# The first four attention units of a fused linear-attention and expert kernel get a program of their own

## The reference

```python
def _attn_ref(r, k, v, w, u):                   # B, H, S, D = 4, 8, 768, 48
    for t in range(S):
        kt, vt, rt, wt = (k[:, :, t], v[:, :, t], r[:, :, t], w[:, :, t])
        cur = np.einsum('bhd,bhe->bhde', u[None] * kt, vt)
        y[:, :, t] = np.einsum('bhd,bhde->bhe', rt, state + cur)
        state = wt[:, :, :, None] * state + np.einsum('bhd,bhe->bhde', kt, vt)

x = y.transpose(0, 2, 1, 3).reshape(3072, 384)
h = x @ w_in                                    # 384 -> 2048
x = (h * np.clip(h + 3.0, 0.0, 6.0) / 6.0) @ w_out
logits = x @ phi                                # 32 slots, 4 for each of 8 experts
# soft mixture: slots = softmax(logits, 0).T @ x; each expert: relu(slots @ w1) @ w2;
# out = softmax(logits, 1) @ slot_out
```

## Time and profile before

| | us |
|---|---|
| median of 3 runs | 466.13 (465.29 to 466.23) |
| the profiled execution | 466.87 |
| its span, first to last instruction | 465.2 |
| first product of a unit | starts at 8.54 |
| first MLP product (s = 0) | starts at 56.84 |
| first MLP product of group 1 (s = 16) | starts at 117.76 |

### The profile page before, as it was taken

How to read it: one execution, slowest core, us unless ns; L and a number is a source line. 1 busy time by engine, 2 the same in 40 slices (tenths; PEclk the granted TensorE clock), 3 DMA queues, 4 the chain that set the end, 5 groups by cost and what they waited for, 6 DMA issues and landing times.

```text
span 465.2 us, 9561 instructions
## 1 busy us (share of the span) xinstructions
PE 429.4 (92%) x3774; PEld 228.5 (49%) x3774; DVE 358.0 (77%) x577; ACT 155.1 (33%) x277; POOL 209.1 (45%) x207
## 2 busy tenths in 40 slices
PE   2977898899999999999999999899999999999974
PEld 1544464545556555655555566355553443443420
DVE  6789989988888888988899989888875576562233
ACT  2234333443334324323435143242333222231122
POOL 5889856456652666456555455655460000000000
PEclk9989999899999999999999999999999999999975
DMA  8999333035812321332233303331006952669729
GB/s 229 277 348 345 89 111 92 20 112 191 281 30 104 111 79 46 101 112 66 54 103 112 112 4 109 110 112 54 1 1 264 408 185 94 236 260 419 306 71 336
DMA packets 16844, 70.91 MB, mean 152 GB/s; under 512 B 2080, under 2 KB 5280, under 8 KB 14752
## 3 DMA queue, kind: packets, MB, share of 16 engines
q1 hardware_dynamic: 16800, 70.30, 44.0%
HBM read 65.57 MB, written 4.72 MB: 151 GB/s over the span
## 4 chain that ended last, share of the span: by engine, by line
PE 49%; issue 21%; DVE 14%; POOL 8%; ACT 5%; DMA 1%; DVEq 0%; SPq 0%; POOLq 0%; ACTq 0%
PE hid L471 6%; PE hid L473 5%; PE hid L472 5%; PE l_ps L527 4%; DVE gated L788 4%; PE hid L489 3%; POOL att L1134 3%; DVE att L738 3%; PE sc_ps L401 3%; POOL att L1144 3%; PE hid L648 2%; PE l_ps L501 2%; PE y_ps L440 2%; POOL att L1128 2%; PE inc_ps L424 2%
## 5 line engine op out<-in xcount | busy, mean ns | idle before, releaser
L471 PE MATMUL hid<-x_split,w_split 128*128 128x512 f16 x288 | 109.9, 381 | 2.6 <-DVE x_split L761 2.6
L472 PE MATMUL hid<-x_split,w_split 128*128 128x512 f16 x288 | 109.6, 381 | 0.0
L473 PE MATMUL hid<-x_split,w_split 128*128 128x512 f16 x288 | 109.6, 380 | 0.0
L1134 POOL TENSOR_TENSOR att<-att 128x512 f16<-128x512 f32 x48 | 59.4, 1237 | 108.1 <-ACT att L993 108.1
L1027 ACT ACTIVATE relu<-hid,three 128x512 f32<-128x512 f32 x96 | 65.7, 684 | 126.7 <-PE hid L473 126.3
L788 DVE SCALAR_TENSOR_TENSOR gated<-relu,hid 128x512 f32<-128x512 f32 x96 | 65.4, 681 | 31.5 <-ACT relu L1027 31.1
L798 DVE STREAM_TRANSPOSE ring<-gated 128x512 f32<-128x512 f32 x96 | 68.3, 711 | 3.3
L993 ACT ACTIVATE att<-att 128x512 f16<-128x512 f32 x48 | 30.3, 631 | 99.0 <-DVE att L738 94.5
L401 PE MATMUL sc_ps<-att 48*128 48x128 f32 x384 | 35.8, 306 | 17.9 <-DVE att L732 8.5
L471 PEld LDWEIGHTS hid<-x_split,w_split 128*128 128x128 f16 x288 | 28.5, 99 | 40.0 <-issue 7.5
L401 PEld LDWEIGHTS sc_ps<-att 48*128 48x128 f32 x384 | 26.5, 195 | 40.6 <-issue 31.1
(11 more groups left out here) (195 smaller groups left out, 763.5 us busy)
## 6 DMA issues: line engine op xcount, KB each, us to landing
att<-nat_dram SPq DMA_DIRECT2D x22, 576.0 KB, 4.1
att<-rkT_dram SPq DMA_DIRECT2D x22, 448.0 KB, 5.5
att<-w_dram SPq DMA_DIRECT2D x5, 1536.0 KB, 14.3
att<-wT_dram SPq DMA_DIRECT2D x22, 226.2 KB, 4.7
out_dram<-w_split SPq DMA_DIRECT2D x24, 192.0 KB, 2.5
stage<-w_in_dram SPq DMA_DIRECT2D x2, 1536.0 KB, 25.1
ring<-w_outT_dram SPq DMA_DIRECT2D x1, 3072.0 KB, 30.0
stage<-w_dram SPq DMA_DIRECT2D x2, 1536.0 KB, 10.3
```

The lines of the kernel that those rows point to most:

```text
L471: pe.matmul(hid[s % 2][:], high, x_high, start=(q == 0), stop=False)
L472: pe.matmul(hid[s % 2][:], high, x_low, start=False, stop=False)
L473: last = pe.matmul(hid[s % 2][:], low, x_high, start=False, stop=(q == KT - 1))
L1134: nc.gpsimd.tensor_tensor(halves(scores_lo, half), halves(scores, half), halves(scores_hi, half), ALU.subtract).then_inc(scores_lo_done, 1)
```

## The change

The head of steps with s < 0 is gone. Each engine has a written-out program for units 0 to 3 and part of unit 4, and then the loop from s = 0.

- **Units 0 to 3:** no fp16 split of scores and v. `mask_first` masks both halves, and `attend_first` multiplies the masked fp32 scores by fp32 v: 8 products instead of 24.
- **Diagonal:** GpSimd multiplies the r and k rows once (`multiply_rows`), TensorE sums over the head dimension with u as a matrix of 2 columns (`diagonal`, 4 products), ScalarE copies the result (`copy_diag`). Units from 4 on keep the old way.
- **Loads:** of `nat`, units 0 to 3 load v alone (192 KB), in a new order below; a small array `u_blocks` is loaded beside `u`.
- **Start:** TensorE opens with 16 products of zeros. State memsets on GpSimd come after unit 0's keys and first product; the fp16 copy of the identity moves to ScalarE; `make_fold` (16 copies at s = 5) becomes 4 copies at the start.
- **Around s = 0:** unit 4's `turn_keys`, `increment`, `attend` and all of `weigh_phi` come after the first MLP step; `high_w` and `low_w` of a piece come one or two steps later. VectorE turns the product of phi at s = 3.

```diff
@@ SP
             for n in range(B):
                 load_rows(n)
-                load_nat(n)
                 if n == 0:
-                    sp.dma_start(u_all, u.rearrange("h d -> (h d)").partition_broadcast(P)).then_inc(u_in, 16)
-            load_w_in(0)
+                    sp.dma_start(u_rows[0:PD, :], u_blocks).then_inc(u_rows_in, 16)
+                load_values(n)
+                if n == 2:
+                    load_w_in(0)
             load_rows(B)
             sp.dma_start(phi_sb[:], phi).then_inc(phi_in, 16)
+            sp.dma_start(u_all, u.rearrange("h d -> (h d)").partition_broadcast(P)).then_inc(u_in, 16)
+            load_nat(B)
             sp.dma_start(w_outT_stage, w_outT).then_inc(w_outT_in, 16)
-            load_nat(B)
+            load_rows(B + 1)
+            load_nat(B + 1)
             load_w_in(1)
@@ TensorE
+            def attend_first(n):
+                if n:
+                    pe.wait_ge(x_lo_done, n)
+                pe.wait_ge(nat_in[n % B], 16)
+                for p in range(PB):
+                    if p % 2 == 0:
+                        pe.wait_ge(masked, 2 * n + p // 2 + 1)
+                    for j in range(2):
+                        cols = slice((2 * p + j) * D, (2 * p + j + 1) * D)
+                        last = pe.matmul(y_ps[:, cols], scores[:, (j * PB + p) * P:(j * PB + p + 1) * P],
+                                         nat_of(n, 2)[:, cols], start=True, stop=True, skip_group_check=True)
+                last.then_inc(y_ready, 1)
...
+            for _ in range(16):
+                pe.matmul(hid[0][:, :], warm[:, 0:P], warm[:, P:P + GT], start=True, stop=True, skip_group_check=True)
+            for half in range(2):
+                score(0, half, None)
+            pe.wait_ge(pool_consts, 2)
+            pe.wait_ge(ident16_done, 1)
+            diagonal(0)
+            for n in range(B):
+                if n:
+                    for half in range(2):
+                        score(n, half, None)
+                turn_keys(n)
+                if n + 1 < B:
+                    diagonal(n + 1)
+                else:
+                    stay_warm(2, hid[0])
+                attend_first(n)
+                increment(n, None)
+                turn_x(n)
+                stay_warm(1, hid[0])
+            for half in range(2):
+                score(B, half, None)
@@ VectorE
+            make_fold()
+            scan_suffix(0)
+            restart_prefix(0)
+            scan_prefix(0)
+            decay_receptance(0)
+            for n in range(B):
+                scan_suffix(n + 1)
+                restart_prefix(n + 1)
+                if n:
+                    low_x(n - 1)
+                mask_first(n)
+                scan_prefix(n + 1)
+                finish_y(n)
+                decay_receptance(n + 1)
+            low_x(B - 1)
+            low_w(0)
+            mask_first(B)
+            low_v(B)
+            sum_diag(B)
```

More of the change, by code:

```diff
@@ L46, with build_program @@
 LAST_INC = UNITS - B
-def build_program(nc, wT, rkT, nat_in_dram, u, w_in, w_outT, w_out, phi, w1, w2, out):
+def build_program(nc, wT, rkT, nat_in_dram, u, u_blocks, w_in, w_outT, w_out, phi, w1, w2, out):
     with ExitStack() as ctx:
@@ L204, in build_program @@
         u_in = sem("u_in")
+        u_rows_in = sem("u_rows_in")
         phi_in = sem("phi_in")
@@ L420, in increment @@
                 pe.wait_ge(nat_in[n % B], 16 * (n // B + 1))
-                if s >= FT and s % FT == 3:
+                if s is not None and s >= FT and s % FT == 3:
                     pe.wait_ge(logits_done, s // FT)
@@ L445, in attend @@
                         there = slice((2 * p + j) * D, (2 * p + j + 1) * D)
-                        pe.matmul(c, scores_hi[:, here], v_hi[n % 2][:, there], start=not from_state, stop=False,
+                        pe.matmul(c, scores_hi[:, here], v_hi[n % 2][:, there], start=False, stop=False,
                                   skip_group_check=True)
@@ L740, in mask_scores, with mask_first @@
                                         ALU.mult).then_inc(masked, 1)
+            def mask_first(n):
+                dve.wait_ge(scores_ready, 4 * n + 4)
+                if n:
+                    dve.wait_ge(y_ready, n)
+                for half in range(2):
+                    nc.vector.tensor_tensor(halves(scores, half), halves(sc_ps[:, :], half),
+                                            mask[:].rearrange("p (o n) -> p o n", o=1).broadcast_to([P, 2, 2 * P]),
+                                            ALU.mult).then_inc(masked, 1)
             def finish_y(n):
@@ L891, in _ @@
                         sum_diag(n)
+                if s == 0:
+                    gate(0)
+                    turn_gated(0)
+                    low_w(1)
+                    scan_suffix(B + 1)
+                    restart_prefix(B + 1)
                 if phase == 3:
@@ L1165, in _ @@
             nc.gpsimd.memset(ident[:], 0.0).then_inc(ident_step, 1)
-            for b in range(B):
-                last = nc.gpsimd.memset(state[b], 0.0)
-            last.then_inc(pool_consts, 1)
             pool.wait_ge(ident_step, 1)
@@ L1181, in _ @@
             nc.gpsimd.memset(three[:], 3.0 * GATE).then_inc(pool_consts, 1)
-            nc.gpsimd.tensor_copy(ident16_sb[:], ident[:]).then_inc(pool_consts, 1)
-            for s in range(FIRST, END):
+            decay_keys(0)
+            multiply_rows(0)
+            for b in range(B):
+                last = nc.gpsimd.memset(state[b], 0.0)
+            last.then_inc(state_zeroed, 1)
+            multiply_rows(1)
+            for n in range(B):
+                decay_keys(n + 1)
+                diag_values(n)
+                if n + 2 < B:
+                    multiply_rows(n + 2)
+            decay_state(B)
+            diag_products(B)
+            for half in range(2):
+                low_scores(B, half)
+            diag_values(B)
+            decay_keys(B + 1)
+            for s in range(END):
                 n, phase = unit_of(s)
-                in_head = n + 1 < HEAD
                 if phase == 0 and is_unit(n):
```

200 lines of the change are left out of this document (122 added, 78 removed).

## The result

| | before | after | forecast |
|---|---|---|---|
| median of 12 executions each | 466.51 | 461.58 | 450.1 |
| lowest to highest | 465.29 to 469.55 | 452.02 to 466.83 | 445 to 457 |
| ratio, with interval | | 0.974 [0.9708, 0.9771] | 0.966 |

The changed kernel is faster, but its executions differ by 14.8 us where those of before differ by 4.3. The ratio leaves out executions over 1.5% above the fastest of a kernel, which are 7 of the 12 after; those kept have a median of 455.21. By the ratio the change saves 2.6%, 12.1 us, where 16.0 was forecast; by the medians of all 12 it saves 4.9. So the side was right and the size was not: 5 of 12 executions lie inside the range, 7 above it.

A forecast was written before the change was run, and what follows sets the result against it. VectorE and GpSimd blocking each other were taken to bound the head, a chain the rest. Terms of -19.7, +4.5 and -0.75 gave -16.0 us, 466.87 to 450.9, median 450.1; range 445 to 457.

The forecast's parts named there:

- TensorE's part of a unit: Head, units 0 to 3: TensorE's scores, small groups and `attend_first` cost nothing unless the clock is low.
- the first rival: Head: TensorE falls to the lower clock, a unit's path gains 2.4 us, two units make 455; chance 0.17.
- Start: Head's opening: first scan at 3.5 us instead of 4.02, receptance product done at 8.05 against 8.39, almost no gain.
- Unit 0 to 1: Head: hangs on GpSimd's row products, state memsets, keys and diagonal values; receptance of unit 1 at 17.1, 9.0 us.
- `attend_first`: Units 0 to 3 on TensorE: fp32 products taken at 1.5 us, between 0.7 and 2.8.
- Loads: DMA into the head: at 226 GB/s each need is covered, by 1 to 3 us; `w_outT` in at 36 to 37.
- Loads as the bound: Rival, head: loads of values in short rows cost 4.5 us, unit 3's keys come 3 to 4 late, 454; chance 0.17.
- MLP to unit 5's mask: From first MLP product to unit 5's first mask: 12.3 us instead of 7.81, a loss of 4.5.
- Group 0: Behind unit 5's first mask: fold copies gone, phi transpose and one more `low_w` added, net -0.75 us.
- Locks hide fully: Rival, head: VectorE and GpSimd locks hidden, a unit takes 5.3 us, four units save 3 more, 447; chance 0.13.
- Slower than before: Rival: TensorE stays at 1.2 GHz into group 0, all 16 steps make about 473 us; chance 0.03.
- No gain: Rival: group 0's chain holds its dates by something other than unit 5's mask, such as weights; chance 0.02.

The follow-up runs named there:

- five more products in the lull: Changed kernel plus five padding products in unit 0, where TensorE waits for GpSimd's second row product: median 452.13 us, ratio 0.9708.
- full loads: The five and two version, with units 0 to 3 loading the whole of `nat` instead of v alone: 457.36 us, ratio 0.976.
- four behind each unit: Changed kernel with four padding products behind each of units 0 to 3 instead of one: median 456.52 us, ratio 0.9768.
- fold back: Changed kernel with the fold's 16 copies back after step 5, none at the start, one execution: first masks of units 5 and 6 18.39 us apart, not 16.64.
- changed kernel again: Changed kernel, nothing edited, run again as a control on the chip of later runs: median 454.85 us, ratio 0.9746.
- five and two: Changed kernel plus five padding products in unit 0's TensorE wait for GpSimd, and two behind each unit instead of one: median 451.58 us, ratio 0.9664.
- early memsets: The five and two version with state memsets ahead of unit 0's keys: 458.23 us with two products in unit 0's wait, 459.22 with five.
- no opening: Changed kernel without the 16 opening products of zeros on TensorE: median 455.43 us, ratio 0.9743.

## Why the prediction was right and wrong

**Side and mechanism: right.** The head before was paced by the two engines that block each other: without its padding and at half of TensorE's speed its units moved only from 9.7 to 10.1. The change took that away. With the level kept up for most of the head, the dates are those of the forecast: first MLP product at 37.4 (forecast 37.1), receptance of units 1 to 4 ready at 16.3, 22.3, 29.2 and 35.6 (17.1, 23.4, 29.2, 35.4), unit 5's first mask at 49.15 (49.4), unit 8's at 97.21 (about 97), group 1's first MLP product at 102.05 (about 102), span 449.7 (449.2). These are of the kernel with five more products in the lull, not of the changed kernel as it stands. That they fit to a few tenths is in part luck: units 1 and 2 came 0.8 and 1.1 us early, and the dip at 20 us took it back, with 6.9 us from unit 2 to unit 3 for a forecast 5.8.

**The step that failed** is the pricing of TensorE's part of a unit: "So it costs nothing unless the clock is low", and in the first rival "At the lower level a unit's path gains 1.1 on the scores and about 1.3 on attend and turn_x, 2.4". I followed a path through TensorE and never added up its whole unit. That sum is 5.70 us without a gap at the full level, next to VectorE's 5.8 in my forecast, and 10.60 at the lower one. So the new plan has two bounds at nearly the same height at 2.4 GHz, and at 1.2 GHz TensorE alone is the bound: 4.9 us more a unit, twice the 2.4 priced. In the profiled execution `attend_first` of units 0 to 3 stands at 13.19, 23.79, 34.39 and 43.58; with five products in the lull at 12.60, 18.81, 26.04 and 31.75. It loses 0.6, 5.0, 8.4 and 11.8. The first MLP product is then 49.18 - 37.44 = 11.7 us late and the span 461.6 - 449.7 = 11.9 longer. The mean clocks say the same: 0.949 over 461.6 us is 2 x 0.051 x 461.6 = 47 us at half speed, 0.982 over 449.7 us is 16; the 31 us between cost 11.9.

**The chance that failed** is 0.17 for this rival against 0.48 for the forecast. Each profile of the changed kernel or of a variant of its head has at least one stretch at the low level; in two it is only the dip at 20 us. I argued with the 57 padding products that were to go. What should have weighed more is that the padded head of before didn't hold the level either: its mean clock is 0.96, and it has a score group of 1.15 us instead of 0.71:

```profile
31.31 1.15 PE L401 MATMUL sc_ps<-att 48*128 48x128 f32 x8
```

The row at 84.30 is of a fall after 2.60 us of idle; I used it for the price, not for the chance. The rival's 455 for two units is too low as a price; that it equals the 455.21 above is luck.

**Terms, one by one.**
- *Start.* First scan at 3.58 (3.5), receptance product done at 7.8 (8.05), scores at 7.96: right.
- *Unit 0 to 1*, 9.0 on GpSimd: memsets and row product did stand ahead of the keys as forecast. The values ended at 14.46 instead of 15.2. At the full level receptance follows at 16.27 after 7.82, 8.4 us. There GpSimd was not alone: its values ended at 14.48, and `finish_y` at 14.60 waited for `attend_first`.
- *`attend_first`*, taken at 1.5 between 0.7 and 2.8: 1.96, and 3.63 at the low level.
- *Loads.* Right that they are covered, wrong in the rate: 350 to 409 GB/s from 8.5 to 37 us, not 226. `w_outT`, issued at 18.79, took 14.4 us and was in at 33.2 instead of 36 to 37. The 226 from the earlier trace rows counts only what was issued up to unit 3's `nat`. In the same 17.54 us of before the DMA engines moved more, with their share as high as here:

```profile
7.06:24.60 17.54, 14.80 (x100) 9.27 (x101) 13.63 (x18) 6.70 (x12) 13.12 (x10) 1.00 1.04 287
```

Why they move more still in the new head isn't shown. Loads as the bound (0.17): refuted for the changed kernel, real with full loads. Its 4.5 us for three loads of values should read 4.3, three times 2.3 less 0.87.
- *MLP to unit 5's mask*, 12.3: 49.15 - 37.44 = 11.7 at the full level, 60.88 - 49.18 = 11.7 in the profile of after.
- *Group 0*, -0.75: mask 5 to mask 8 takes 48.06, against 48.27 before, so -0.2. The fold's term is shown (1.75). The stretch from unit 5 to 6 is 16.64 where 17.46 - 1.72 + 0.3 = 16.0 was forecast, and 6 to 7 and 7 to 8 are 15.71 each for a forecast 15.74. The 0.6 between isn't traced to one instruction.
- *Locks hide fully* (447): not seen, no execution of the changed kernel is below 452.02. *Slower than before*: two executions, 466.66 and 466.83, reach the median of before, so the clock can eat the whole gain; the level is 1.00 in group 0 though, which is what that rival needed to fall. *No gain*: refuted, masks move with the head.

**Open.** What makes the level fall or hold isn't settled, and the lull at 11 us explains less than the experiments with padding suggest. The level rises somewhere within the 16 opening products (each takes 0.63 us at first and 0.38 at the end), not at the same date in each execution. In the two profiles of the changed kernel:

```profile
1.32 5.48 PE L577 MATMUL hid<-logits 128*128 128x512 f16 x16 [1.32 <-DVE logits L927]
```

```profile
1.32 6.21 PE L577 MATMUL hid<-logits 128*128 128x512 f16 x16 [1.32 <-DVE logits L927]
```

The shorter the opening products, so the sooner the level had risen, the sooner it fell again:

| profile | opening products, us | five in the lull | first fall, us |
|---|---|---|---|
| full loads | 4.93 | yes | 10.8 |
| four behind each unit | 5.04 | no | 11.0 |
| changed kernel | 5.48 | no | 11.9 |
| fold back | 5.80 | no | 12.6 |
| changed kernel again | 6.21 | no | 13.4 |
| five in the lull | 6.22 | yes | 20.3 |
| five and two | 6.40 | yes | 20.6 |

Only the last three have openings of like length. Among them the five products put the fall off by 7 us; with an opening of 4.93 they did not. So the rival, that the date of the rise decides much of what I put down to the lull, is untested, and it may be why executions of one kernel differ. In the two versions with early memsets the level fell at 9.8 and 9.3, inside idle of 2.61 and 2.83 us. And a fall needs no gap: besides those at 20.3 and 20.6, it came at 30.3 (no opening), 31.5 (four behind each unit) and 29.7 (fold back), with TensorE busy without a gap for more than 9 us ahead of each. The profiles are of one execution each.

## What to carry to other kernels

Add up each engine's whole work of a unit, not only its part of the path, and do it at both levels of TensorE's clock: a plan that takes the bound from slow engines puts it on the next one, and if that is TensorE the kernel inherits its clock. Products that look like padding are worth little while another engine sets the pace (before: 16 opening ones added, 1.0011; all 57 of the head taken out, 1.0045) and are worth something once it doesn't (five and two: 451.58 against 454.85 on one chip). Before a stall is moved off one engine, look at what starts later through it: the early memsets put the first scan off by 1.2 us, the first scores by 2.1, and lost the level.

## What the hardware showed

- The granted clock fell to 0.50 at 11.9 us after 1.00 us of waiting, and in five other profiles with TensorE busy 1.00 of 1.00: at 20.3 and 20.6 us, with no idle over 0.39 since the scores of unit 0, and at 29.7, 30.3 and 31.5 us with none in the 9 us ahead. It stayed at 0.50 for 30.6 us of products without a gap, nearly all fp32, and rose again within them.
- The first fall came later the later the level had risen in the opening products: openings of 4.93, 5.04, 5.48, 5.80 and 6.21 us went with falls at 10.8, 11.0, 11.9, 12.6 and 13.4.
- The clock column shows 1.00 until the first change of level, also where products take twice their time (scores 1.23 for 0.71 over the whole head).
- Four small copies on VectorE took 2.08 instead of 0.91 beside memsets on GpSimd, and a prefix scan 2.10 instead of 1.23 beside a product there.
